# First block of a fused linear-attention and two-layer network kernel: other PSUM places for y, wider selection products, one weight load behind the repack, another order on GpSimd

## The reference

```python
for t in range(S):
    kt, vt, rt = (k[:, :, t], v[:, :, t], r[:, :, t])
    cur = np.einsum('bhd,bhe->bhde', u[None] * kt, vt)
    y[:, :, t] = np.einsum('bhd,bhde->bhe', rt, state + cur)
    state = w[None, :, :, None] * state + np.einsum('bhd,bhe->bhde', kt, vt)
...
x = y as (3072, 384)
h = np.maximum(x @ w_in, 0.0);  x2 = (h * h) @ w_out        # 384 -> 2048 -> 384
out = ((x2 @ w_a) * (x2 @ w_b)) @ moe2_w_out                # 384 -> 1536 -> 384
```

## Time and profile before

| | |
|---|---|
| median of 3 runs | 917.19 us (916.93 to 918.1) |
| the profiled execution | 917.79 us, of which its span 916.0 us |
| busy in the span | PE 906.1 us (99%), DVE 389.8 (43%), ACT 285.9 (31%), POOL 122.7 (13%) |
| granted TensorE clock | 0.999 on average |

### The profile page before, as it was taken

How to read it: one execution, slowest core, us unless ns; L and a number is a source line. 1 busy time by engine, 2 the same in 40 slices (tenths; PEclk the granted TensorE clock), 3 DMA queues, 4 the chain that set the end, 5 groups by cost and what they waited for, 6 DMA issues and landing times.

```text
span 916.0 us, 16503 instructions
## 1 busy us (share of the span) xinstructions
PE 906.1 (99%) x6951; PEld 775.1 (85%) x6951; DVE 389.8 (43%) x600; ACT 285.9 (31%) x501; POOL 122.7 (13%) x125
## 2 busy tenths in 40 slices
PE   8999999999999999999999999999999999999997
PEld 6888888888888888888888888888888888888887
DVE  8778665546555555336542212322321222222122
ACT  3534433333333233345542222212222222222121
POOL 7355422232223221000000000000000000000000
PEclk9999999999999999999999999999999999999999
DMA  9987545636435320043330001002002002001001
GB/s 150 172 145 145 94 66 107 92 77 86 79 65 94 56 61 20 18 135 116 91 108 1 1 13 58 1 1 70 0 1 69 1 1 69 1 1 32 3 1 35
DMA packets 175736, 53.39 MB, mean 58 GB/s; under 512 B 147885, under 2 KB 174126, under 8 KB 175662
## 3 DMA queue, kind: packets, MB, share of 16 engines
q1 hardware_dynamic: 168640, 47.22, 25.6%
q10 hardware_dynamic: 7022, 5.12, 2.4%
HBM read 38.54 MB, written 9.44 MB: 52 GB/s over the span
## 4 chain that ended last, share of the span: by engine, by line
PE 96%; SPq 2%; DMA 0%; DVE 0%; issue 0%; ACT 0%
PE banks L853 11%; PE banks L855 11%; PE banks L854 11%; PE banks L739 8%; PE banks L723 7%; PE banks L740 7%; PE banks L743 7%; PE banks L725 7%; PE banks L724 7%; PE banks L867 5%; PE banks L871 5%; PE banks L868 5%; PE banks L641 1%; PE banks L654 1%; PE banks L621 1%; PE banks L664 1%
## 5 line engine op out<-in xcount | busy, mean ns | idle before, releaser
L1304 DVE TENSOR_TENSOR g_raw<-banks,g_raw 128x512 f32<-128x512 f32 x72 | 49.8, 692 | 277.0 <-PE banks L855 277.0
L853 PE MATMUL banks<-xT,weights 128*128 128x512 f32 x360 | 140.2, 389 | 0.0
L854 PE MATMUL banks<-xT,weights 128*128 128x512 f32 x360 | 140.0, 389 | 0.0
L855 PE MATMUL banks<-xT,weights 128*128 128x512 f32 x360 | 140.0, 389 | 0.0
L739 PE MATMUL banks<-g_hi,weights 128*128 128x512 f32 x288 | 114.8, 398 | 0.0
L723 PE MATMUL banks<-xT,weights 128*128 128x512 f32 x288 | 112.4, 390 | 0.8 <-DVE xT L1201 0.8
L1188 DVE TENSOR_TENSOR g_lo<-banks,g_hi 128x512 fp32r<-128x512 f32 x94 | 65.0, 692 | 112.7 <-ACT g_hi L915 112.7
L740 PE MATMUL banks<-g_hi,weights 128*128 128x512 f32 x288 | 112.2, 390 | 0.0
L724 PE MATMUL banks<-xT,weights 128*128 128x512 f32 x288 | 112.1, 389 | 0.0
L725 PE MATMUL banks<-xT,weights 128*128 128x512 f32 x288 | 112.0, 389 | 0.0
L915 ACT ACTIVATE g_hi<-banks 128x512 fp32r<-128x512 f32 x94 | 56.3, 599 | 148.3 <-PE banks L743 109.0
(11 more groups left out here) (131 smaller groups left out, 1247.8 us busy)
## 6 DMA issues: line engine op xcount, KB each, us to landing
rkv<-in_v SPq DMA_DIRECT2D x24, 192.0 KB, 4.5
x_dram<-stage SPq DMA_DIRECT2D x6, 768.0 KB, 3.5
xT<-x_dram SPq DMA_DIRECT2D x6, 768.0 KB, 5.4
result<-stage SPq DMA_DIRECT2D x22, 192.0 KB, 3.0
xT<-y_pad SPq DMA_DIRECT2D x22, 144.0 KB, 2.8
stage<-in_moe_w_out SPq DMA_DIRECT2D x16, 192.0 KB, 3.4
rkv<-in_k SPq DMA_DIRECT2D x12, 192.0 KB, 3.6
rkv<-in_k SPq DMA_DIRECT2D x24, 96.0 KB, 3.6
```

The costliest lines, as they stand in the source:

```text
L853: nc.tensor.matmul(dst, hi, xT[:, q, HI, kt, :], start=(kt == 0), stop=False)
L854: nc.tensor.matmul(dst, hi, xT[:, q, LO, kt, :], start=False, stop=False)
L855: last = nc.tensor.matmul(dst, lo, xT[:, q, HI, kt, :], start=False, stop=(kt == KT - 1))
```

## The change

Units 2 and 3 get y in the bank pairs that units 0 and 1 had, so their `mix_state` no longer has to follow the masks of their own scores; it waits for the copy of y of unit 0 or 1. The new states of units 2 and 3 go to banks 4 and 7, into columns 256 on and 0 on, and are taken in two instructions each. The order of TensorE's products changes, and a filler product of 512 columns is gone. `place_x` multiplies three tiles at once by `choose_own` (384 columns), and places in banks 0 to 3. `load_weights(1)` on SP and `split_hi(1)` on ScalarE move behind the repack and the split of x. `x_lo(0)` moves from VectorE to GpSimd. GpSimd makes unit 2's diagonal products before unit 3's.

```diff
+        def y_banks(e):
+            return ((4, 5), (6, 7))[e % 2] if e < UNITS else (0, 1)
+
+        def state_place(e):
+            return {2: ((4, 7), PAIRS * T), 3: ((4, 7), 0)}.get(e, (y_banks(e), PAIRS * T))
...
+        def x_lo(eng, e):
+            eng.wait_ge(x_hi_made, e + 1)
...
@@ SyncE
-            for i in range(2):
-                load_weights(sp, i)
+            load_weights(sp, 0)
             repack(sp, 0)
-            for i in range(2, STAGES + 1):
+            for i in range(1, STAGES + 1):
                 load_weights(sp, i)
@@ GpSimd
-            for e in range(2, UNITS):
-                k_times_u(e)
+            k_times_u(2)
+            times_r(2)
             pool.wait_ge(tail_made, 1)
             tail(0)
-            for e in range(2, UNITS):
-                times_r(e)
+            k_times_u(3)
+            times_r(3)
             tail(1)
...
             decay(2)
+            x_lo(pool, 0)
             decay(3)
@@ TensorE, mix_state
-                pe.wait_ge(masked, e + 1)
+                if e < UNITS:
+                    pe.wait_ge(y_made, e - 1)
+                else:
+                    pe.wait_ge(masked, e + 1)
@@ TensorE, place_x
+                    y, to = y_part(y_in, e), placed(e, part)
+                    nc.tensor.matmul(to, choose_own[0:PR], y[:, 0:KT, :], start=True, stop=False)
                     for kt in range(KT):
-                        to, y = placed(e, part)[:, kt, :], y_part(y_in, e)
-                        nc.tensor.matmul(to, choose_own[0:PR], y[:, kt, :], start=True, stop=False)
-                        last = nc.tensor.matmul(to, choose_last[kt][0:PR], y[:, KT, :], start=False, stop=True)
+                        last = nc.tensor.matmul(to[:, kt, :], choose_last[kt][0:PR], y[:, KT, :], start=False,
+                                                stop=(kt == KT - 1))
@@ TensorE, the prologue's order
             score(3)
+            mix_state(2)
             pe.wait_ge(y_made, 2)
             renew_state(1)
-            pe.wait_ge(state_made, 1)
-            warm_long(bank[5])
-            mix_state(2)
+            first_scores(2)
             mix_state(3)
-            first_scores(2)
             first_scores(3)
@@ ScalarE
-            for i in range(2):
-                split_hi(act, i)
+            split_hi(act, 0)
             take_y(2)
...
-            for i in range(2, STAGES + 1):
+            for i in range(1, STAGES + 1):
                 split_hi(act, i)
@@ VectorE, keep_state
-                dve.wait_ge(mixed, e + 1)
+                dve.wait_ge(mixed, e + 2 if e == 2 else e + 1)
...
+                elif e < UNITS:
+                    dve.wait_ge(decay_made, e - 1)
+                    for i in range(2):
+                        last = nc.vector.tensor_tensor(to[:, i, :], bank[pair[i]][0:PR, at:at + PAIRS * D],
+                                                       kept_part[:, i, :], ALU.add)
@@ VectorE, the prologue's order
+            sum_diagonal(2)
             for e in range(2, UNITS):
                 scale_r(e)
-            sum_diagonal(2)
             keep_state(0)
             sum_diagonal(3)
+            mask(2)
             keep_state(1)
-            mask(2)
             mask(3)
...
-            for e in range(2):
-                x_lo(e)
             for e in range(2, UNITS):
                 first_x_lo(e)
+            x_lo(nc.vector, 1)
```

More of the change, by code:

```diff
@@ L200, in placed @@
         def placed(e, part):
-            return bank[2 * e + part][:, 0:DM].rearrange("p (k t) -> p k t", k=KT)
+            return bank[2 * (e - 2) + part][:, 0:DM].rearrange("p (k t) -> p k t", k=KT)
         def matrix_of(e):
@@ L390, in split_lo @@
             last.then_inc(w_lo_made, 1)
+        def x_lo(eng, e):
+            eng.wait_ge(x_hi_made, e + 1)
+            q, cols = e // UNITS % 2, cols_of(e)
+            eng.tensor_tensor(xT[:, q, LO, :, cols], xT[:, q, LO, :, cols].bitcast(F32),
+                              xT[:, q, HI, :, cols].bitcast(F32), ALU.subtract).then_inc(x_lo_made, 1)
         def store_last(eng, p, i):
@@ L626, in y @@
                 row = (q ^ i) * HP
-                return bank[banks_of(e)[i]][row:row + n, g * T:(g + 1) * T]
+                return bank[y_banks(e)[i]][row:row + n, g * T:(g + 1) * T]
             def mix_state(e):
-                pe.wait_ge(masked, e + 1)
+                if e < UNITS:
+                    pe.wait_ge(y_made, e - 1)
+                else:
+                    pe.wait_ge(masked, e + 1)
                 pe.wait_ge(state_made, kept(e - 1))
@@ L659, in renew_state @@
                 pe.wait_ge(k_tail_made, e + 1)
+                pair, at = state_place(e)
                 for g in range(PAIRS):
@@ L662, in renew_state @@
                         rows, h = slice(i * T, (i + 1) * T), 2 * g + (q ^ i)
-                        at = PAIRS * T + g * D
-                        last = nc.tensor.matmul(bank[banks_of(e)[i]][q * HP:q * HP + D, at:at + D],
+                        last = nc.tensor.matmul(bank[pair[i]][q * HP:q * HP + D, at + g * D:at + (g + 1) * D],
                                                 k_tail[rows, e % 2, 2 * g + q, :],
@@ L923, in take_y @@
                     act.wait_ge(mixed, e + 1)
-                y = both(banks_of(e), 0, PAIRS * T)[0:PR].rearrange("p i (g t) -> p i g t", g=PAIRS)
+                y = both(y_banks(e), 0, PAIRS * T)[0:PR].rearrange("p i (g t) -> p i g t", g=PAIRS)
                 to = y_part(g_hi, e) if 2 <= e < UNITS else y_pad[0:PR, :, e % 2 * P:(e % 2 + 1) * P]
@@ L1171, in keep_state @@
                 to = state[0:PR, first_batch:first_batch + 2, :, :].rearrange("p i g d -> p i (g d)")
-                new = both(banks_of(e), PAIRS * T, PAIRS * D)[0:PR]
+                kept_part = decayed[0:PR].rearrange("p i g d -> p i (g d)")
+                pair, at = state_place(e)
                 if e < 2:
-                    nc.vector.tensor_copy(to, new).then_inc(state_made, 1)
+                    last = nc.vector.tensor_copy(to, both(pair, at, PAIRS * D)[0:PR])
+                elif e < UNITS:
[3 more added lines that the diff above has]
+                                                       kept_part[:, i, :], ALU.add)
                 else:
                     dve.wait_ge(decay_made, e - 1)
-                    nc.vector.tensor_tensor(to, new, decayed[0:PR].rearrange("p i g d -> p i (g d)"), ALU.add)\
-                        .then_inc(state_made, 1)
+                    last = nc.vector.tensor_tensor(to, both(pair, at, PAIRS * D)[0:PR], kept_part, ALU.add)
+                last.then_inc(state_made, 1)
             def square(n, f):
@@ L1201, in first_x_lo @@
                 nc.vector.tensor_copy(xT[:, 0, LO, :, cols_of(e)], placed(e, LO)).then_inc(x_lo_made, 1)
[L1203 to L1208, removed]
             def x2_lo(n, kt):
@@ L1252, in layer1 @@
                     for e in beside[SPLIT].get(s, []):
-                        x_lo(e)
+                        x_lo(nc.vector, e)
                     if n == LAST and 8 <= f < 8 + KT:
```

## The result

The changed kernel takes 921.57 us in the median of 6 runs (919.53 to 923.63), the kernel before 917.6 us on the same chip: a ratio of 1.0039, 95% interval 1.0021 to 1.0056. I had forecast 916.0 us and no change that can be told; 914.5 to 917.9 was the range. The profiled run took 920.1 us, span 918.4 us, 2.4 us more than before.

A forecast was written before the change was run, and what follows sets the result against it. TensorE's work was taken as the bound from the first layer product on. A start 2.4 us earlier, less 1.3 us returned as a hole, gave 1.1 us gain: median 917.19 to 916.0 us, range 914.5 to 917.9.

The forecast's parts named there:

- From the first layer product on the kernel is TensorE's work alone, which the change leaves as it is.: From 29.4 us on TensorE is busy for 870.5 of 870.6 us; only that stream's start or a new hole can matter.
- The filler lay in a wait and is worth nothing itself: TensorE's prologue: dropping the 512-column filler product neither gains nor costs time.
- fourth rival: Without the filler TensorE's clock falls from 2.4 to 1.2 GHz in the prologue, up to 4 us: 919 to 921; chance 0.03.
- The prologue's order: TensorE's new order before the layers: last scores product ends at 22.9 instead of 24.49 us, 1.6 us earlier.
- The wide products: Selection products in the prologue: 12 narrow and 4 of 384 columns take 2.1 us, 0.7 less than before.
- The repack: SP's repack DMAs: last one starts between 21.7 and 23.5 us, letting `up(0, 0)` start at about 27.0 instead of 29.41.
- The hole ahead of `up(0, 2)`: TensorE waits about 1.3 us for the relu behind weights 3, landed at 31.2; `up(0, 2)` at 32.5; chance 0.56.
- third rival: Weights 3 land after 32.3, `up(0, 2)` 0.9 to 1.5 us later than 33.62: 918.1 to 918.7 us; chance 0.13.
- second rival: The excess came from weights 1 in SP's queue and goes with them; 2.4 us earlier, 914.6 to 915.3 us; chance 0.25.
- the excess: Extra time of SP's long DMA issues, 2.3 us before; read as issues standing still beside instruction fetches, 1.4 us left.
- holes further on: Sign of a wrong prediction: TensorE idle later, at `down(0, 0)` or where unit 4 is turned; no size given.

The follow-up runs named there:

- ten fewer: The kernel before with wide selection products and no filler product, ten TensorE matmuls fewer, SP's order as before: 919.09 us, ratio 1.0024.
- two tiny transposes: The kernel before without its filler product, the instruction count restored by two tiny transposes at the start: 918.43 us, ratio 1.0015.
- The DMA part alone: The kernel before with weights 1 behind the repack on SP and ScalarE, wide selection products and eight tiny transposes: 918.78 us, ratio 1.0011.
- five transposes: The changed kernel with five tiny 4x4 transposes ahead of `up(0, 0)`, without a filler: 918.79 us, ratio 1.002.

## Why the prediction was wrong

*"From the first layer product on the kernel is TensorE's work alone, which the change leaves as it is."* This step failed. The change leaves the work and takes 20 instructions away ahead of it (ten matmuls with their weight loads), and that moved the ends of the instruction blocks. The stream comes in blocks: the page of before has 55 packets on queue q8, 0.90 MB, so 16.4 KB each, for 13,902 matmuls and weight loads, 253 for each packet.

```profile
q8 instruction: 55, 0.90, 0.4%
```

A group of small products uses up 256 instructions in 1.9 us. In the kernel before a fetch lies in the window from 61 to 65.9 us, ahead of the group; after, it begins at the group's end. The DMA view's instruction rows, of before (61 to 65.9) and of after (67.9 to 70.3):

```profile
q8 instruction: 1, 0.02, 1.2%
```

```profile
q8 instruction: 1, 0.02, 2.3%
```

No row of q8 stands in the window from 57 to 68 us of after (two small packets of q14 do). Cost 1.9 us by the profile. Shown by giving the instructions back (ten: the stop is gone), by taking them from the kernel before (its own stop), and by the stop in the prologue, which moves by as many passes as are put ahead of it: 28, 26, 24, 18 for 0, 2, 4, 10. The packet times agree: in all 13 stops, in ten traces, TensorE resumed 1.3 to 1.5 us after its q8 packet ended (20.76 and 22.05, 68.98 and 70.33 in the first profile), and in the ten traces without the stop near 68 us the packet began 3.1 to 3.7 us ahead of the group, in the four with it 1.6 to 1.9 us behind the group's start. What sets off a packet stays open: measured against the group, that one came 5.5 us later in the changed kernel, where ten matmuls are 2.3 us of work, and with five or six matmuls fewer than before it moved by less than 0.4 us. I had read the fetches as something that holds SP's queue, and had not asked whom they feed. The Trainium skill's section that I cited (Runtime: NRT & Kernel Launch, Instruction fetch mechanics) gives blocks of 256 instructions fetched while the block before runs; the rows agree with the size, by the 253 above. Its "mostly hidden" does not hold at these two places, which cost 0.81 and 1.73 us.

*"The filler lay in a wait and is worth nothing itself"*, and the fourth rival's chance of 0.03. Wrong by 2.7 us in half of the 12 runs: so far the six with the low clock lie above the four whose clock held, in the median; 2.9 to 3.9 in the other kernels without the filler. My argument, that the new order has less idle time, was made from the order and missed the stop in `renew_state(1)`. Without the filler 31 of 75 runs had a mean clock of 0.992 to 0.994 (the changed kernel, its variants, and the kernel before without it); with it 2 of 56 (variants), and none of the 93 runs of the kernel before. The chips differ between the rounds, but on one chip it was 8 of 24 against 1 of 23, on another 8 of 12 against 1 of 33. The four profiles of such runs show a stop of 1.35 to 2.06 us and the clock at half from 22.5 to 23.2 us on, until 32.7 to 36.5; with a stop of 0.81 us it held, and with stops of 1.41 and 1.42 us and the filler beside them too. Without the filler a wait of 1.36 us for a state ended once with the clock at half from 23.1 to 26.5 us (ten fewer) and once without a fall (two tiny transposes). It is the filler that matters, but what exactly tips the clock in one run and not in the next stays open.

*The prologue's order.* The last scores product ended at 24.6, not at 22.9. The stop of 0.81 us is half of the 1.7. The rest is a path that I had wrong: I had unit 3's state product ahead of the last mask, but it needs `keep_state(1)`, and that waits for `renew_state(1)`.

```profile
22.39 0.56 DVE L1190 COPY state<-banks 112x384 f32<-112x384 f32 x1 [1.50 <-PE banks L681]
```

So `mix_state(3)` could start only at 23.10, and the 0.69 us of unit 3's scores follow it, not the mask. The wide products cost about 0.50 us a group (26.29 to 26.80), as said.

*The repack* was right: its last issue started at 22.46, between 21.7 and 23.5. `up(0, 0)` came at 28.59 instead of 27.0, for VectorE's sake.

*The hole ahead of `up(0, 2)`* was right: 0.84 us where 1.3 was said, released by the relu, which stood behind weights 3. But its place was mis-sized: the last DMA of weights 3 was issued 0.56 us later than forecast and took 3.94 us to land instead of 3.4, so it landed at 32.30 and not at 31.2. The 1.1 us of gain at `up(0, 2)` went with that, whatever `up(0, 0)` did: it is the third rival's side, which begins at a landing of 32.3. The DMA part alone shows the same mechanism at full size, 1.40 us. *The second rival*, that the excess goes with weights 1, failed: at the last issue some 2.0 us of the 2.3 of excess were left, where I had taken 1.4. The reading of the excess, an issue that stands still beside a fetch, fits every trace: in all 14 the two longest issues that SP began between 18 and 28 us end 0.31 to 0.40 us after a q8 packet has ended, the one of 2.49 us with a packet of 2.10 us and the one of 1.55 with one of 1.17. (Behind 30 us there are issues as long with no such packet.)

In sum: 0.2 us (prologue, forecast -1.1), 1.9 us (the stop), and 1.5 us more in the median, which goes with the clock: 3.6 of the 4.0 measured. The prediction had named holes further on as a sign that it is wrong, but gave them no price. Without the stop near 68 us and with the clock held the changed kernel is back at about the time of the kernel before, as the seven runs with five transposes show: 917.0 to 918.9. The gain of 1.1 us that was forecast shows in no version.

## What to carry to other kernels

Count TensorE's instructions, not only its time: a burst of small matmuls used up a fetched block in 1.9 us here, and removing ten matmuls with their weight loads far ahead put the end of a block where the fetch had no cover. When a wait is released by nothing that the profile shows, look whether it stays at the same instruction count as instructions are added in front. And price a filler by what happens in several runs, each with its mean clock, not by the wait in which it lies.

## What the runs showed of the hardware

The stop in the prologue was 0.81 us in one run and 2.06 us in another of the same program up to there; it ended 1.3 to 1.5 us after the instruction packet each time, so it is long where the packet starts late (20.97 us with 2.06) or takes long (1.54 us with 1.48). The two longest DMA issues that SP began between 18 and 28 us (0.9 to 2.5 us, most others there took 0.4 to 0.7) ended 0.31 to 0.40 us after such a packet, in all 14 traces. Ten 4x4 transposes made a kernel of 922.4 us 4.4 us faster in the median. And two kernels in which a product with start set went to columns 256 to 511 of a PSUM bank, while y of unit 2 stood unfinished in columns 0 to 255, had their output off by 0.064; with the filler in bank 6 it was not. That the start disturbed the unfinished sum is inferred from this; which values were off is not known.
